# Attention by head on halves of the TensorE array, with the queries transposed by VectorE

## The reference

```python
# attention, for each batch and head: no softmax
kv  = einsum('bhsd,bhse->bhde', k, v)            # 64 x 64 per head
out = einsum('bhsd,bhde->bhse', q, kv)           # 576 x 64 per head
x   = out / sqrt(mean(out*out, -1) + 1e-6) * g_norm
x   = heads side by side                         # 576 x 512 per batch
# second block
theta = x @ w_theta
y = w_tok_r @ (x*cos(theta)) + w_tok_i @ (x*sin(theta))   # over tokens
u = x + y
x2 = u + relu(u @ w_ch)
# third block: two more token matrices, then 512 -> 1536 -> 512 with relu
```

## Time and profile before

| | |
|---|---|
| median of three runs | 1215.68 us (1215.0 to 1219.2) |
| profiled execution | 1213.61 us, of it 1211.8 us span |
| TensorE busy | 1182.7 us, 98% |
| VectorE busy | 836.4 us, 69% |
| ScalarE busy | 490.0 us, 40% |
| GpSimd busy | 338.2 us, 28% |
| granted TensorE clock | 0.995 of full, mean |

### The profile page before, as it was taken

One profiled execution on the slowest core, in us unless ns is written; L12 is line 12 of the kernel. 1 busy time (PEld: TensorE's weight loads), 2 busy tenths in 40 slices (PEclk: granted clock), 3 DMA queues, 4 the chain that ended last, 5 costly groups with the idle time before them and its releaser, 6 DMA issues.

```text
span 1211.8 us, 20530 instructions
## 1 busy us (share of the span) xinstructions
PE 1182.7 (98%) x7590; PEld 1150.9 (95%) x7590; DVE 836.4 (69%) x1227; ACT 490.0 (40%) x764; POOL 338.2 (28%) x209
## 2 busy tenths in 40 slices
PE   6999999999999999999999899999999999999998
PEld 5899999999999999999898899999999899999998
DVE  3877778686868778678556566766766786666664
ACT  3532424242433324244433455555556543333331
POOL 4443534444252525440553042133210000000000
PEclk9999999999999999999999999999999999999999
DMA  9825445272543440036998587856669999989973
GB/s 254 172 53 112 79 94 101 39 156 39 111 76 86 78 107 10 34 87 227 344 300 295 164 332 267 298 201 263 248 233 334 382 304 300 271 240 308 290 189 53
DMA packets 348428, 228.12 MB, mean 188 GB/s; under 512 B 268880, under 2 KB 316368, under 8 KB 347344
## 3 DMA queue, kind: packets, MB, share of 16 engines
q1 hardware_dynamic: 348368, 227.32, 64.7%
HBM read 136.84 MB, written 92.80 MB: 189 GB/s over the span
## 4 chain that ended last, share of the span: by engine, by line
PE 91%; DMA 3%; DVE 2%; issue 1%; ACT 1%; SPq 1%; POOL 0%; DVEq 0%; POOLq 0%; ACTq 0%
PE bank L42 11%; PE bank L44 11%; PE bank L43 11%; PE bank L1267 10%; PE bank L1269 10%; PE bank L1268 10%; PE bank L309 6%; PE bank L314 6%; PE bank L308 6%; PE bank L240 3%; PE bank L265 3%; PE bank L279 1%; PE bank L253 1%; DMA attention_g<-g_scratch 1%; DMA qkv_x_tokens<-x_tokens_scratch 1%
## 5 line engine op out<-in xcount | busy, mean ns | idle before, releaser
L308 PE MATMUL bank<-weights_tok,z_z 128*128 128x288 f32 x576 | 164.2, 299 | 0.0
L309 PE MATMUL bank<-weights_tok,z_z 128*128 128x288 f32 x576 | 161.3, 295 | 0.0
L314 PE MATMUL bank<-weights_tok,z_z 128*128 128x288 f32 x576 | 124.8, 294 | 0.0
L309 PEld LDWEIGHTS bank<-weights_tok,z_z 128*128 128x128 f32 x576 | 108.2, 188 | 0.0
L308 PEld LDWEIGHTS bank<-weights_tok,z_z 128*128 128x128 f32 x576 | 108.1, 188 | 0.0
L838 POOL TENSOR_TENSOR weights_rms_inverse<-weights_mean_squares,weights_minus_half 128x8 f32<-128x8 f32 x40 | 65.5, 1639 | 129.6 <-DVE weights_mean_squares L632 129.3
L314 PEld LDWEIGHTS bank<-weights_tok,z_z 128*128 128x128 f32 x576 | 92.6, 188 | 0.0
L519 ACT ACTIVATE weights_x_channel_major<-attention_u 128x288 fp32r<-128x288 f32 x64 | 28.4, 444 | 139.4 <-DVE attention_u L699 138.8
L853 POOL TENSOR_TENSOR z_z<-tokens_cos,z_z 128x512 fp32r<-128x512 f32 x24 | 34.5, 1437 | 173.5 <-ACT z_z L512 173.5
L42 PE MATMUL bank<-weights_x_channel_major,weights_ch 128*128 128x288 f32 x256 | 77.2, 301 | 0.0
L43 PE MATMUL bank<-weights_x_channel_major,weights_ch 128*128 128x288 f32 x256 | 75.4, 294 | 0.0
(11 more groups left out here) (287 smaller groups left out, 3697.7 us busy)
## 6 DMA issues: line engine op xcount, KB each, us to landing
g_scratch<-attention_staged SPq DMA_DIRECT2D x36, 960.0 KB, 5.0
weights_g<-g_scratch SPq DMA_DIRECT2D x24, 1152.0 KB, 10.3
g_scratch<-attention_staged SPq DMA_DIRECT2D x36, 384.0 KB, 5.6
x_scratch<-attention_u SPq DMA_DIRECT2D x8, 1152.0 KB, 4.5
u_scratch<-attention_u SPq DMA_DIRECT2D x8, 1152.0 KB, 6.2
weights_raw_u<-u_scratch SPq DMA_DIRECT2D x6, 1536.0 KB, 7.4
qkv_u_left<-u_scratch SPq DMA_DIRECT2D x12, 768.0 KB, 9.4
qkv_k<-in_k_dram SPq DMA_DIRECT2D x32, 256.0 KB, 4.9
```

The source lines that it names most:

```text
L308: pe.matmul(out, x, wtok[0][:, zt, hs], start=(i == 0), stop=False)
L309: pe.matmul(out, x, wtok[1][:, zt, hs], start=False, stop=False)
L314: mm = pe.matmul(tok_bank(b, g)[:, 0:HALF], z[1][:, zt, c * P:(c + 1) * P], wtok[0][:, zt, half * HALF:(half + 1) * HALF], start=False, st ...
```

## The change

Key products are done for one head at a time: 64 weight columns and 64 moving columns, two heads of a pair on the two column halves of the array (their results go to partitions 0 to 63 and 64 to 127). The result has no unwanted blocks, one copy brings it to `kv_heads`. Query products are done for one head at a time too: 64 rows of weights (the head's 64 channels of a block of 128 queries) and 64 moving columns, the two heads of a pair on the two row halves, into two different banks of a pair of banks (`ps_heads`).

TensorE no longer transposes queries and ScalarE no longer copies them. The queries are loaded as 32 x 32 blocks (16 DMAs a batch of 128-byte pieces, in place of 5), and VectorE transposes within blocks, four instructions of 128 x 576 a batch, to get all of a batch's queries with channels on partitions. VectorE does this for batch 0 at the start, for batch 1 in `body(0)` behind the rotations, and for batch b + 2 at the end of `body(b)`, for b from 0 to 5. The loads of batch 0's queries are issued from ScalarE's queue, the others from SyncE's ahead of the keys and values.

Buffers move: `square` lies in `fraction`, the second `x_normed` lies over `x_left`, which brings a wait for all theta products in front of the sines of tile 3; `x_transpose` of tiles 0 and 1 waits for norm 3. The order of VectorE for batch 0 changes: `x_lo(0, 0)` and `x_lo(0, 1)` stand behind all norms.

```diff
+    def load_q(eng, n):
+        wait(eng, d_q, HP * n)
+        for hp in range(HP):
+            for part in range(PARTS):
+                h, first = 2 * hp + part // 2, part % 2 * SIDE
+                eng.dma_start(q_raw[part * SIDE:(part + 1) * SIDE, hp, :].rearrange("p (b d) -> p b d", d=SIDE),
+                              q[n, h, :, first:first + SIDE].rearrange("(b s) d -> s b d", s=SIDE)
+                              ).then_inc(s_q, DMA)
...
         def body(b):
+            load_q(sp, b + 2)
             load_kv(b + 2)
-            load_q(b + 2)
             store(b)
...
         def kv(n):
...
                 for hp in range(HP):
-                    hs = slice(2 * hp, 2 * hp + 2)
-                    mm = pe.matmul(ps_kv[:, hp * P:(hp + 1) * P], kin[:, j, hs, :].rearrange("p h d -> p (h d)"),
-                                   vin[:, j, hs, :].rearrange("p h d -> p (h d)"), start=(j == 0 and hp == 0),
-                                   stop=(j == NT - 1 and hp == HP - 1))
+                    for side in range(2):
+                        h = 2 * hp + side
+                        mm = pe.matmul(ps_kv[side * D:(side + 1) * D, hp * D:(hp + 1) * D], kin[:, j, h, :],
+                                       vin[:, j, h, :], start=(j == 0 and hp == 0),
+                                       stop=(j == NT - 1 and hp == HP - 1))
...
-        def q_transpose(n, j):
...
         def attend(n, j):
-            pe.wait_ge(a_qt, NT * n + j + 1)
-            pe.wait_ge(d_kv, 2 * (n + 1))
+            pe.wait_ge(d_q, HP * (n + 1))
+            pe.wait_ge(d_kv, n + 1)
...
             for hp in range(HP):
-                mm = pe.matmul(ps_out[j % 2][:, hp * P:(hp + 1) * P], qt[:, j % 2, hp, :], kvbd[:, hp, :],
-                               start=True, stop=True)
+                for side in range(2):
+                    hs = slice(side * D, (side + 1) * D)
+                    first = hp * S + j * P
+                    mm = pe.matmul(ps_heads[j % 2][:, side, hp * D:(hp + 1) * D],
+                                   qt[hs, first:first + P], kv_heads[hs, hp, :], start=True, stop=True)
             mm.then_inc(p_out, 1)
 
         def x_transpose(n, j):
             pe.wait_ge(g_x, NT * n + j + 1)
-            if j == 1:
-                pe.wait_ge(a_qt, NT * (n + 1))
+            if j < 2:
+                pe.wait_ge(d_xn, NT * n + NJ)
...
             if more:
                 kv(b + 1)
-                q_transpose(b + 1, 0)
...
         def sines(b, j):
...
+            if j == NJ - 1:
+                act.wait_ge(p_theta, NT * (b + 1))
...
+        load_q(act, 0)
         act.wait_ge(s_ident, 4)
...
         def kv_copy(n):
...
-            dve.tensor_copy(kvbd[0:D, :, 0:D], pv[0:D, :, 0:D]).then_inc(d_kv, 1)
-            dve.tensor_copy(kvbd[D:P, :, D:P], pv[D:P, :, D:P]).then_inc(d_kv, 1)
+            dve.tensor_copy(kv_heads[:, :, :], ps_kv[:, 0:HP * D].rearrange("p (a e) -> p a e", a=HP)).then_inc(d_kv, 1)
+
+        def turn_q(n):
+            dve.wait_ge(s_q, HP * PARTS * DMA * (n + 1))
+            wait(dve, p_out, NT * n)
+            for hp in range(HP):
+                dve.transpose(qt[:, hp * S:(hp + 1) * S], q_raw[:, hp, :]).then_inc(d_q, 1)
...
         kv_copy(0)
+        turn_q(0)
 
         mean_square(0, 0)
         mean_square(0, 1)
...
+        norm(0, 4)
         x_lo(0, 0)
...
         x_lo(0, 1)
-        norm(0, 4)
...
+            if first:
+                turn_q(1)
             if more:
                 kv_copy(b + 1)
...
                 for j in range(1, NT):
                     x_lo(b + 1, j)
                 turn_x2(b, NC - 1, turned)
+                if turn:
+                    turn_q(b + 2)
```

More of the change, by code:

```diff
@@ L107, in phase_a @@
     ps_out = banks[2:4]
+    ps_heads = [bank_pairs[1], bank_pairs[0]]
     ps_acc = banks[4:8]
@@ L118, in phase_a @@
     s_kv, s_q, s_store = sem("a_ld_kv"), sem("a_ld_q"), sem("a_store_x2")
-    s_kv0, s_q0 = ([sem(f"a_ld_kv0_{j}") for j in range(NT)],
-                   [sem(f"a_ld_q0_{j}") for j in range(NT)])
+    s_kv0 = [sem(f"a_ld_kv0_{j}") for j in range(NT)]
     s_raw = [sem(f"a_ld_raw{i}") for i in range(5)]
@@ L181, in load_kv @@
                 load_tile(vin, v, n, j, s_kv)
-        def load_q(n):
-            wait(sp, p_qt, NT * n)
-            for j in range(NT):
-                load_tile(qin, q, n, j, s_q)
         def store(n):
@@ L476, in squares @@
             wait(act, d_ss, NT * n + j)
-            act.activation(square[:, :], ps_out[j % 2][:, :], ACT.Square).then_inc(a_sq, 1)
+            act.activation(square.rearrange("p (s c) -> p s c", s=2), ps_heads[j % 2][:, :, 0:HP * D],
+                           ACT.Square).then_inc(a_sq, 1)
         def x_hi(n, j):
@@ L750, in vector, with body @@
         tok_weight_lo(3)
+        norm(0, 2)
+        mean_square(0, 3)
+        tok_weight_lo(4)
         theta_weight_lo(0)
-        mean_square(0, 3)
-        norm(0, 2)
-        tok_weight_lo(4)
+        norm(0, 3)
+        mean_square(0, 4)
+        theta_weight_lo(1)
+        norm(0, 4)
         x_lo(0, 0)
-        theta_weight_lo(1)
-        mean_square(0, 4)
-        norm(0, 3)
         x_lo(0, 1)
-        norm(0, 4)
-        def body(b, first=False, more=True):
+        def body(b, first=False, more=True, turn=True):
             if first:
@@ L828, in vector @@
         body(0, first=True)
-        loop(dve, body, 1, B - 1)
+        loop(dve, body, 1, B - 2)
+        body(B - 2, turn=False)
         body(B - 1, more=False)
@@ L2031, in build @@
         m["x_out"] = [m[f"x_out{i}"] for i in range(10)]
-        banks = [ctx.enter_context(nc.psum_tensor(f"bank{i}", [P, 512], F32)) for i in range(8)]
-        a = phase_a(ctx, nc, m, banks, q, k, v, g_norm, w_theta, w_tok_r, w_tok_i, w_ch, x2_dram, x2t_dram)
+        bank_pairs = [ctx.enter_context(nc.psum_tensor(f"banks{i}", [P, 2, 512], F32)) for i in range(4)]
+        banks = [bank_pairs[i // 2][:, i % 2, :] for i in range(8)]
+        a = phase_a(ctx, nc, m, banks, bank_pairs, q, k, v, g_norm, w_theta, w_tok_r, w_tok_i, w_ch, x2_dram, x2t_dram)
         b = phase_b(ctx, nc, m, banks, a["done"], a["store_last_turned"], x2_dram, x2t_dram, w_tok1, w_tok2, w_ch1, u2_dram)
```

109 lines of the change are left out of this document (36 added, 73 removed).

## The result

The changed kernel takes 1234.85 us (median of 4 runs, 1233.6 to 1239.08) against 1215.83 (4 runs) for the kernel before: a ratio of 1.0157, 95% interval 1.0126 to 1.0188. It is slower, by 19 us; the forecast was 1227. The profiled execution took 1234.56 us, its span 1232.8, 21.0 more than the 1211.8 before.

A forecast was written before the change was run, and what follows sets the result against it. The prediction took TensorE, at 98% of the span, as the bound. Its terms, -12.5 + 0 + 9.6 + 6.4 - 1.3 + 10 = +12.2 us on 1213.6, gave 1225.8, forecast as a 1227 us median, range 1204 to 1270.

The forecast's parts named there:

- the likeliest case: The main forecast for the whole kernel: 1227 us, its own range 1215 to 1240, chance 0.36.
- Query transposes, -12.5: Token mixing, batches 1 to 7: four query transposes of 0.445 us each leave TensorE per batch, -12.5 us.
- Query products, no change: Query tiles on TensorE: 16 half-array pairs with loads side by side take 0.89 us a tile, no change.
- Drain, +9.6 in 0 to 19: Array changes between whole and halves around query products: 35 tiles at 0.27 us, +9.6 us, range 0 to 19.
- Four transposes at the end of a batch, +1.06 each: VectorE's batch-end transposes delay theta product 2 and mixing: +1.06 us, six times, +6.4 us.
- Batch 0, -1.3: Batch 1's query turn falls where VectorE has room; batch 1's shorter key products give -1.3 us.
- Head, +10 in 5 to 13: Kernel start: query loads, transposes and later theta product 0, less about 1 us, +10 us, range 5 to 13.
- The last batch, -0.4: From the last batch's key products on: -1.78 us for query transposes, +1.35 for array changes.
- (a): Rival: row halves load one behind another; +41 us without drains, 1257, or 1266 with drains; chance 0.24.
- (d): Rival: halves run as a whole array would, pairs still 0.111 us; 1287 us; chance 0.06.
- (c): Rival: half-row loads take half the stream too, query products 0.45 us a tile; 1197 us; chance 0.14.
- (b): Rival: halves are free, no drain, head only +5; -3.7 us, 1212, no change that can be told; chance 0.20.

The follow-up runs named there:

- e7: Every query product computed twice into the same place, against the changed kernel: 1273.14 us, 1.0477 of the kernel before.
- e1: VectorE's four block transposes moved from the batch's end into channel mixing, one each, against the changed kernel: 1225.99 us, 1.0086 of the kernel before.
- e6: Key products whole with two copies of the diagonal blocks, query products still by head, against the changed kernel: 1237.96 us, 1.0188 of the kernel before.
- e2: In batch 0, batch 1's query turn and key-value copy moved earlier on VectorE, against the changed kernel: 1230.31 us, 1.0127 of the kernel before.
- e3: x_lo(0, 0) put ahead of norm(0, 4) in batch 0, against the changed kernel: 1233.67 us, 1.0151 of the kernel before.
- e9: e4 plus unread identity products where TensorE waits in batch 0's head: 1213.88 us, 0.9993 of the kernel before.
- e4: The edits of e1, e2 and e3 together, against the changed kernel: 1218.02 us, 1.0020 of the kernel before.
- e8: Batch 0's query loads put behind key and value loads on SyncE's queue, against the changed kernel: 1234.22 us, 1.0157 of the kernel before.
- e11: e4 with query products on the whole array against a block-diagonal matrix, key products still on column halves: 1207.26 us, 0.9941 of the kernel before.
- e10: The kernel before with only its key products by head on column halves: 1213.13 us, 0.9982 of the kernel before.
- e5: Key and query products reordered so all heads of one array half precede the other's, against the changed kernel: 1255.4 us, 1.0331 of the kernel before.
- e12: e11 plus e9's unread identity products in batch 0: 1205.48 us, 0.9923 of the kernel before.

## Why the prediction came out as it did

The sign was right, and 1234.85 lies in the likeliest case's own range of 1215 to 1240, 8 us over its value. (The last addition had a slip: 1225.8 and 2.1 are 1228.) The mechanism was right for the full batches: +0.63 forecast for each, +0.78 measured, by the waits that were named. It was not for the start of the kernel: the head cost 14.1 where the range was 5 to 13, and batch 0 cost 6.1 where I had a small gain. Together they are 20.2 of the 21.0 us, and the forecast had 9.3 there. That the total still fell into the range is in part luck, since 2.0 us came off in a stretch that the change doesn't touch. By its steps:

- **Query transposes, -12.5.** Right as a gross sum: 0.44 us a tile is what the trace lost.
- **Query products, no change.** Right: 0.892 for 16 pairs (e7), loads side by side. Key products were put at 2.3 and took 2.48. That the loads "never overlap" in the trace before was a misreading: they last 0.19 us and start 0.108 apart.
- **Drain, +9.6 in 0 to 19.** Mis-sized a little. Measured 0.34 a tile, 35 x 0.34 = 11.9. At the first tile of batch 3 the load of the first pair starts 0.223 us behind the start of the last mixing product and the first mixing load 0.200 behind the last pair, where in a run of mixing a load starts beside the product before it. The Trainium skill, TensorEngine Tiling (Array Packing), Key Properties, says that changing the mode drains the array and that different tiles load and multiply in parallel. The trace after agrees with both, with 0.34 us more a tile for its two changes and loads 7 ns apart. That is less than the 0.55 that I had put for two full drains.
- **Four transposes at the end of a batch, +1.06 each.** Right in place, and nearly in size. They take 2.71 (forecast 2.76), the stall is 1.86 by the stages (12.87 us for the theta products of the four full tiles against 11.01; forecast 2.2), and the saving of 2.34 on key products and the first transpose is mostly given back at mixing, 1.32 us for GpSimd. Together 1.86 - 2.34 + 1.32 = +0.84. e1 shows the first part and e6 the last.
- **Batch 0, -1.3.** This step failed: "the turn of batch 1's queries comes after the chain, where VectorE has room". VectorE had idled 2.5 us for ACT there and had 2.29 us of a weight split before the turn; TensorE already stood idle 2.56 us at that place in the kernel before, which I had not read. With 2.71 more on VectorE it stood 4.99, and its clock showed 0.50 from 87.2 to 93.8. The query tile and the 27 mixing products from 88.69 on took 7.17 us, and the next such group 4.83, so the slow clock cost 2.3. The stretch cost +6.1 where I had -0.7 in all. e2 took 5.9 of it back.
- **Head, +10 in 5 to 13.** Too low by 4, and outside its range. Up to the first query product I was too pessimistic: 23.53 against a forecast 25, +5.4 where I had +7. From there to theta product 0 the kernel before takes 14.62 us and the changed one 21.84, +7.2 where I had +3.3; this term was mis-sized. From theta product 0 to batch 1's key products it is +1.6, which I had at nothing. The record of the clock is missing there, but the theta products last 0.63 us there, against 0.39 later on, and query tiles 1.97 against 1.11; in e6, whose trace has the record, the stretch from 25 to 50 us is at 0.50, and the kernel before shows 1.00 at that place. I had priced the head as an offset at a given speed, not as a wait with a slower array behind it. Of the 7.2, the order is 2.2 (e3), and 1.9 goes with the idle products (e9), as do the 1.6 behind (1.5 in e9). What the other 3 are no run takes apart.
- **The last batch, -0.4.** -1.3: no turn stands ahead of it, and I had left out its shorter key products. Another -2.0 lies in the stages behind attention, which the change doesn't touch. It goes with the clock of the one execution that was profiled. The kernel before has two stretches at half the clock in these stages, the changed kernel one:
```profile
603.30:606.50 3.20, 3.20 (x16) 3.20 (x15) 2.88 (x7) 0.69 (x1) 2.04 (x1) 0.50 1.10 266
968.50:971.70 3.20, 3.20 (x11) 3.20 (x11) 3.20 (x2) 1.21 (x1) 0.00 (x0) 0.50 1.02 387
```
```profile
626.50:629.70 3.20, 3.20 (x15) 3.20 (x15) 2.93 (x6) 0.92 (x1) 1.80 (x1) 0.50 1.06 256
```
From the last batch's key products to the end, the five traces with no such stretch (e4, e6, e8, e9, e11) take 747.4 to 749.1 us, the seven with one 749.1 to 753.3, the two with two (the kernel before and e10) 754.0 and 754.1. No run isolates it, and TensorE was busy throughout these stretches.

Of the rivals, (a) and (d) fell to the loads 7 ns apart and to e7, (c) to the same 0.892, and (b) to the 0.34 us a tile for changes and to the head.

## What to carry to other kernels

A change that takes work off the bounding engine is worth what the next waits leave of it: here 1.9 us saved in one place came out as 0.55 to 0.9, since another engine's input was due 12 us later, and the stages of one period, read from product to product, show that before any run. Before putting work in a place "with room", look at what stands ahead of it on that engine and whether the bounding engine already waits there; a short wait that grows may cost its own length, and slow work may stand behind it. Use halves of the array where whole stages run on them, as the 80 key products do, and keep whole products where the mode would change again every few multiplies.

## What the runs showed of the hardware

- Two halves of the array share one stream's time only while neighbouring instructions alternate. Grouped by half, three or four instructions get ahead and a tile costs 1.53 us in place of 1.03 (e5).
- A change from whole to halves and back costs 0.34 us in all at full clock, 0.17 a change on average (16 pairs among 27 mixing products; how it divides between the two the rows don't say).
- After an idle 2.56 us TensorE went on at full clock in the kernel before. At the same place the granted clock was 0.50, 1.2 GHz, around and behind an idle 2.79 us (e10, 72.9 to 79.7) and 4.99 us (the changed kernel, 87.2 to 93.8). After an idle 1.42 us it stayed full in e2; after 1.41 at the same place it fell in e4. So the length of the wait alone doesn't decide it, and what does no run here shows. It was also 0.50 in stretches of the last stages in which TensorE had no gap.
- In the head the clock was 0.50 in e6 (25 to 50 us), 0.78 with products in the waits (e9, 25 to 48) and 0.78 in e11 without them, 0.93 with both (e12).
